# A delta-rule attention and two gated networks on one core: the inverse spread evenly, four array quadrants, spaced loads, one block

## The reference

```
attention, per batch and head:      kt = k / (|k| + 1e-6), state = 0 (48 x 48)
  for t in 0..767:                  y[t] = q[t] @ state
                                    state += beta[t] * outer(kt[t], v[t] - state.T @ kt[t])
x  = y as 3072 x 384
network 1:                          h = x @ w_in (384 x 2048)
                                    g = 0 if h <= -1, h if h >= 1, else (h + 1)^2 / 4
                                    x2 = g @ w_out (2048 x 384)
network 2:                          xn = x2 / sqrt(mean(x2^2) + 1e-6) * rms_g
                                    out = (silu(xn @ w_gate) * (xn @ w_val)) @ w_out2     (hidden width 1536)
```

## Time and profile before

| | |
|---|---|
| median of 3 runs | 1338.87 us |
| the profiled execution, its own time | 1335.86 us |
| its span, first to last instruction | 1334.1 us |
| PE busy | 1197.8 us, 90% |
| DVE busy | 608.3 us, 46% |
| ACT busy | 430.6 us, 32% |
| mean granted TensorE clock | 0.941 |
| data moved | 47.97 MB, 36 GB/s over the span |

### The profile page before, as it was taken

How to read it: one execution, slowest core, us unless ns; L and a number is a source line. 1 busy time by engine, 2 the same in 40 slices (tenths; PEclk the granted TensorE clock), 3 DMA queues, 4 the chain that set the end, 5 groups by cost and what they waited for, 6 DMA issues and landing times. The chain is left out here.

```text
span 1334.1 us, 24559 instructions
## 1 busy us (share of the span) xinstructions
PE 1197.8 (90%) x10980; PEld 959.9 (72%) x10980; DVE 608.3 (46%) x987; ACT 430.6 (32%) x709; POOL 9.6 (1%) x20
## 2 busy tenths in 40 slices
PE   2597779977998799789979999799999999999997
PEld 2376557755776577567757777688888888888886
DVE  3912860468258625942792244544233232423322
ACT  2333332223433433243234345452222323222211
POOL 1000000000000000000000000000000000000000
PEclk8878975988999899999999999899999999999999
DMA  7604000130022004100100022220101001010101
GB/s 192 142 3 97 0 1 1 27 94 1 2 50 71 2 2 73 47 2 2 49 24 2 2 93 73 75 91 0 48 0 48 0 24 24 0 24 0 24 0 24
DMA packets 18130, 47.97 MB, mean 36 GB/s; under 512 B 2224, under 2 KB 9008, under 8 KB 17456
## 3 DMA queue, kind: packets, MB, share of 16 engines
q1 hardware_dynamic: 18032, 46.51, 13.5%
HBM read 37.06 MB, written 9.44 MB: 35 GB/s over the span
## 5 line engine op out<-in xcount | busy, mean ns | idle before, releaser
L1012 DVE TENSOR_TENSOR pr<-g,vps 128x512 f32<-128x512 f32 x72 | 49.5, 688 | 252.5 <-ACT g L962 252.3
L821 PE MATMUL hps<-xh,w1h 128*128 128x512 f32 x288 | 131.7, 457 | 31.4 <-DVE g L676 31.2
L834 PE MATMUL acc<-g1h,w2h 128*128 128x512 f32 x288 | 129.3, 449 | 12.8 <-DVE g1l L683 12.8
L962 ACT ACTIVATE g<-gps 128x512 f32<-128x512 f32 x72 | 43.1, 598 | 272.3 <-PE vps L1080 272.3
L553 ACT ACTIVATE g1h<-g 128x512 fp32r<-128x512 f32 x96 | 60.6, 631 | 190.8 <-DVE g L676 168.9
L821 PE MATMUL hps<-xl,w1h 128*128 128x512 f32 x288 | 119.8, 416 | 1.6 <-issue 1.6
L821 PE MATMUL hps<-xh,w1l 128*128 128x512 f32 x288 | 119.9, 416 | 0.0
L834 PE MATMUL acc<-g1l,w2h 128*128 128x512 f32 x288 | 117.6, 408 | 0.0
L834 PE MATMUL acc<-g1h,w2l 128*128 128x512 f32 x288 | 117.1, 407 | 0.0
L683 DVE TENSOR_TENSOR g1l<-g,g1h 128x512 fp32r<-128x512 f32 x96 | 66.0, 687 | 85.0 <-ACT g1h L553 84.8
L544 ACT ACTIVATE g<-hps,half_c 128x512 f32<-128x512 f32 x96 | 65.4, 681 | 119.6 <-PE hps L821 118.6
(11 more groups left out here) (133 smaller groups left out, 2225.7 us busy)
## 6 DMA issues: line engine op xcount, KB each, us to landing
kqT<-kq SPq DMA_DIRECT2D x12, 768.0 KB, 11.2
v_in<-v SPq DMA_DIRECT2D x6, 768.0 KB, 4.3
k_in<-k SPq DMA_DIRECT2D x6, 768.0 KB, 13.1
x2d<-x2s SPq DMA_DIRECT2D x18, 256.0 KB, 2.2
x2t<-x2d SPq DMA_DIRECT2D x6, 768.0 KB, 4.3
y<-y_t SPq DMA_DIRECT2D x48, 96.0 KB, 2.2
stage<-w_in SPq DMA_DIRECT2D x4, 768.0 KB, 16.0
stage<-w_out SPq DMA_DIRECT2D x4, 768.0 KB, 4.6
```

What stands on the lines that cost most here:

```text
L821: last = pe.matmul(hps[f % 2][:, :], wt[:, kk, P * f:P * f + P], xx[:, kk, :], start=(kk == 0 and e == 0), stop=(kk == KD - 1 and e == 2))
L834: last = pe.matmul(acc[j][:, :], wt[:, f, P * j:P * j + P], gg[:, f % 2, :], start=(f == 0 and e == 0), stop=(f == NF1 - 1 and e == 2))
L962: act.activation(silu[:, f % 2, :], gps[f % 2][:, :], ACT.Silu).then_inc(e_silu, 1)
L1012: dve.tensor_tensor(pr[:, f % 2, :], silu[:, f % 2, :], vps[f % 2][:, :], ALU.mult).then_inc(e_pr, 1)
```

## The change

It changes six things. (1) The inverse: `DENSE` goes from 690 to 570, `LEAD` from 850 to 700, `GK` of the next step moves ahead of the `KS` groups, so that the inverse of the next step begins earlier in the round; the transposes `tr` and `ft` are three instead of four (one of them over all 128 partitions), and `Z` waits for the first of `ft` alone. (2) The attention's groups cover half of the instances (64 records) instead of a quarter; the small matmuls of `GK`, `GQ`, `KS`, `U`, `QS`, `PU`, `KU` go through all four 64x64 quadrants of the array in turn and write to two banks; `Y` is taken apart into `QS` and `PU`; `Z` and `X` keep their two. (3) The loads: k turned and q turned come separately, k first, and in each round v, k turned, k and q turned are issued after given blocks of network 1. (4) The first part's order: the weight pieces of network 1 are spread over the inverse one by one, and `GQ` of step 1 moves into round 1. (5) Both networks stand in one block; network 2's loops are written out; the last round also prepares network 2's first tile and 15 of its 27 weight pieces, now in single operations of 512 columns; `x2s` is copied by ACT instead of DVE. (6) The sum of squares: DVE adds the three parts (`fold`), and one fp32 matmul is left of three.

```diff
+TURNS = 3
...
 def inversion(c):
-    out = [(("tr", c, qd), 20) for qd in range(P // BLK)] + [(("nrm", c, 0), 14), (("sys", c, 0), 13)]
+    out = [(("tr", c, n), 20) for n in range(TURNS)] + [(("nrm", c, 0), 14), (("sys", c, 0), 13)]
     out += [(("inv", c, s), 4 + (BLK - 1 - s) * (s + 1) // 48) for s in range(INV)]
-    out += [(("ft", c, qd), 20) for qd in (1, 3)] + [(("xd", c, 0), 21)] + [(("ft", c, qd), 20) for qd in (0, 2)]
-    return out + [(("vn", c, 0), 17)]
+    return out + [(("ft", c, 0), 20), (("xd", c, 0), 21)] + [(("ft", c, n), 20) for n in range(1, TURNS)] + [(("vn", c, 0), 17)]
 def solve(c):
-    return [("Z", c, q) for q in range(NQ)] + [("X", c, q) for q in range(NQ)]
+    out = [(kind, c, hf) for kind in ("Z", "X") for hf in range(HALVES)]
+    if 0 < c < NSTEP - 1:
+        out += [("GK", c + 1, hf) for hf in range(HALVES)]
+    return out
 def serial(c):
-    more = c + 1 < NSTEP
-    out = []
-    for hf in range(HALVES):
-        a, b = NQH * hf, NQH * hf + 1
-        grams = [[("GK", c + 1, n)] if more else [] for n in (a, b)]
-        out += grams[0] + [("KS", c, a), ("KS", c, b)] + grams[1]
-        out += [("U", c, a), ("U", c, b), ("Y", c, a), ("KU", c, a), ("Y", c, b), ("KU", c, b)]
-    if more:
-        out += [("GQ", c + 1, n) for n in range(NQ)]
+    out = [(kind, c, hf) for hf in range(HALVES) for kind in ("KS", "U", "QS", "PU", "KU")]
+    if 0 < c < NSTEP - 1:
+        out += [("GQ", c + 1, hf) for hf in range(HALVES)]
     return out
...
-LEAD = 850
-DENSE = 690
+        if e[0] == "sys":
+            out += [("GQ", 0, hf) for hf in range(HALVES)]
+        if e[0] == "inv" and e[2] >= 2:
+            out += split(BESIDE * (e[2] - 1) // (INV - 2) - BESIDE * (e[2] - 2) // (INV - 2))
+    out += [("ft", 0, 0), ("Z", 0, 0), ("Z", 0, 1), ("xd", 0, 0)] + split(1)
+    out += [("X", 0, 0), ("X", 0, 1), ("ft", 0, 1), ("ft", 0, 2), ("vn", 0, 0), ("KS", 0, 0), ("QS", 0, 0)] + split(1)
+    out += [("mask", 0, n) for n in range(NQ)]
+    out += [("U", 0, 0), ("GK", 1, 0), ("PU", 0, 0), ("KU", 0, 0), ("GK", 1, 1)] + split(1)
+    ahead = inversion(1)
+    def some(n):
+        return [ahead.pop(0)[0] for _ in range(n)]
+    out += [("KS", 0, 1)] + split(1) + [("QS", 0, 1)] + some(1) + [("U", 0, 1)] + split(2) + some(2)
+    out += [("PU", 0, 1), ("KU", 0, 1)] + some(2) + split(1) + [("low", 0, NPIECE - 2), ("low", 0, NPIECE - 1)]
+    assert not pieces
+    return out + [("XT", 0, n) for n in range(KD)], ahead
+LEAD = 700
+DENSE = 570
 LAST = 0.90
-EDGE = 0.985
...
-        at += w / LEAD
+        at += w / (LEAD if k == 1 else DENSE)
     lead = at
+    if k == 1:
+        ev += [(0.02 + 0.04 * hf, ("GQ", 1, hf)) for hf in range(HALVES)]
     us = solve(k) + serial(k)
-    span = sum(2 if u[0] == "Y" else 1 for u in us)
-    done, begin = 0, None
-    for u in us:
-        ev.append((lead + (LAST - lead) * done / span, u))
-        done += 2 if u[0] == "Y" else 1
-        if u == ("GK", k + 1, NQ - 1):
-            begin = lead + (LAST - lead) * (done + 1) / span
+    begin = None
+    for n, u in enumerate(us):
+        ev.append((lead + (LAST - lead) * n / len(us), u))
+        if u == ("GK", k + 1, HALVES - 1):
+            begin = lead + (LAST - lead) * (n + 1) / len(us)
     rest = []
     if k + 1 < NSTEP:
         at = begin
         for e, w in inversion(k + 1):
-            if at < EDGE:
+            if at < 1:
...
+def banks():
+    out, held, at = {}, [None] * NBANK, 0
+    for u in [u for plan in PLANS for u in plan]:
+        if u in FIRST or u[0] not in WIDE + NARROW:
+            continue
+        n = 2 if u[0] in WIDE else 1
+        out[u] = [((at + j) % NBANK, held[(at + j) % NBANK]) for j in range(n)]
+        for j in range(n):
+            held[(at + j) % NBANK] = (u, j)
+        at += n
+    return out
...
+def second_network():
+    norms = {2: ["square"], 3: ["fold"], 4: ["sums", "root"], 6: ["invert"], 7: ["invert"], 8: ["scale"], 9: ["hi"], 10: ["lo"]}
+    parts = {0: (15, 17), 1: (17, 19), 2: (19, 20), 3: (20, 21), 4: (21, 22), 5: (22, 24), 6: (24, 26), 7: (26, 27)}
+    out = []
+    for n in range(NSTEP):
+        for f in range(NF2):
+            out.append(("gv", n, f))
+            if f:
+                out.append(("y", n, f - 1))
+            elif n:
+                out += [("y", n - 1, NF2 - 1), ("out", n - 1, 0)]
+            out.append(("silu", n, f))
+            if n == 0:
+                for kind in ("w2h", "w2l"):
+                    out += [(kind, n, p) for p in range(*parts.get(f, (0, 0)))]
+            if n + 1 < NSTEP:
+                out += [(kind, n + 1, int(f == 7)) for kind in norms.get(f, [])]
+    return out + [("y", NSTEP - 1, NF2 - 1), ("out", NSTEP - 1, 0)]
...
+                elif kind == "fold":
+                    dve.wait_ge(e_sq, n + 1)
+                    dve.tensor_tensor(x2sq[:, 0, :], x2sq[:, 0, :], x2sq[:, 1, :], ALU.add).then_inc(e_half, 1)
+                    dve.wait_ge(e_half, n + 1)
+                    dve.tensor_tensor(x2sq[:, 0, :], x2sq[:, 0, :], x2sq[:, 2, :], ALU.add).then_inc(e_fold, 1)
...
+                if kind == "sums":
+                    pe.wait_ge(e_fold, n + 1)
+                    if n:
+                        pe.wait_ge(e_pr, (n - 1) * NF2 + 4)
+                    pe.matmul(sums_of(n)[:, :], ones[:, :], x2sq[:, 0, :], start=True, stop=True).then_inc(e_ss, 1)
+                elif kind == "gv":
...
-                    load_kq(0)
+                    load_kq(0, (0,))
                     sp.dma_start(beta_i[:, :, :].rearrange("p c t -> p (c t)"), beta[:, :]).then_inc(s_beta, 16)
+                    sp.wait_ge(s_kq[0][0], 16 * BP)
+                    load_kq(0, (1,))
                     for n in range(NSTAGE):
                         load_w(n)
                     load_v(0)
-                    load_k(0)
                     for n in range(NSTAGE, NCHUNK):
                         load_w(n)
-                    load_kq(1)
+                    load_kq(1, (0,))
+                    load_k(0)
+                    load_kq(1, (1,))
                     sp.dma_start(gain[:, :], rms_g.rearrange("(k p) -> p k", p=P), allow_slow_non_contiguous=True).then_inc(e_gain, 16)
-                    for c in range(NSTEP):
-                        if c + 2 < NSTEP:
-                            load_kq(c + 2)
+                    def after(n, f):
+                        sp.wait_ge(s_h, NF1 * n + f + 1)
+                    for c in range(1, NSTEP):
+                        load_v(c)
+                        if c > 1:
+                            x2_store(c - 2)
                         if c + 1 < NSTEP:
-                            load_k(c + 1)
-                            load_v(c + 1)
-                        if c:
-                            x2_store(c - 1)
+                            after(c - 1, 0)
+                            load_kq(c + 1, (0,))
+                        after(c - 1, 2)
+                        load_k(c)
+                        if c + 1 < NSTEP:
+                            after(c - 1, 4)
+                            load_kq(c + 1, (1,))
+                    x2_store(NSTEP - 2)
...
-                            p0, b0 = BLK * q, BLK * (q % 2)
-                            dve.transpose(sysm[p0:p0 + BLK, :, :],
-                                          gram[p0:p0 + BLK, :, b0:b0 + BLK].rearrange("p i s -> p s i")).then_inc(s_tr, 1)
+                                if c:
+                                    dve.wait_ge(p_x, HALVES * c)
+                            else:
+                                dve.wait_ge(s_tr, TURNS * c + 1)
+                            rows = (slice(0, P), slice(BLK, C), slice(C + BLK, P))[q]
...
+                    BY_ROW_BP = ((0, 0), (1, 1), (0, 1), (1, 0))
+                    BY_ROW_M = ((0, 0), (0, 1), (1, 0), (1, 1))
+                    BY_ROW_S = ((0, 0), (0, 1), (1, 1), (1, 0))
...
                         if kind == "GK":
-                            if q == 0:
-                                pe.wait_ge(s_kq[c % 2], 16 * MEM * (c // 2 + 1))
-                            for j, i in enumerate(insts(q)):
-                                for m in range(MEM):
-                                    r = slice(C * m, C * m + D)
-                                    last = pe.matmul(ps[C * m:C * m + C, C * j:C * j + C], kqT[c % 2][r, i, 0, :],
-                                                     kqT[c % 2][r, i, 0, :], start=True, stop=True)
+                            if hf == 0:
+                                pe.wait_ge(s_kq[0][c % 2], 16 * BP * (c // 2 + 1))
+                            for h in range(H):
+                                for bp, m in BY_ROW_BP:
+                                    r, i = slice(C * bp, C * bp + D), NPAIR * hf + H * m + h
+                                    last = pe.matmul(bank_of(u, bp)[C * m:C * m + C, C * h:C * h + C], kqT[c % 2][r, 0, i, :],
```

(36 more changed lines are left out.)

766 lines of the change are left out of this document (366 added, 400 removed).

## The result

The changed kernel takes 1111.16 us (median of 4 runs, 1107.6 to 1114.05), the kernel before beside it 1340.78: ratio 0.830, 95% interval 0.8255 to 0.8345. I had predicted 1170.

The account below looks back on a forecast made before the run. PE bounds the kernel: network 2 without gaps, the rounds with waits on DVE and lost clock. First part 86, rounds 618, change of block and network 2 463.5 give 1167.5 span; forecast 1170, own range 1145 to 1195, overall 1095 to 1220.

Parts of the forecast that it names:

- Step "quadrants": Small attention matmuls: four quadrants leave a record at 29.4 ns, set by its columns of weights, so no gain.
- the other end: Same matmuls: each quadrant loads by itself, half price a record, -63 us in the rounds; first rival, 1102 us, chance 0.27.
- The rest of the rounds: Five rounds with network 1: group boundaries, GQ, sum of squares and remaining waits bring 722.4 us to 618.
- Group boundaries: Rounds: groups of 64 records instead of 32 leave out 66 boundaries of 0.33 us, -21.8 us.
- Waits left: Rounds: PE's remaining waits and lost clock, 15 us in round 1, 6 in round 2, 4 in each other, +33.
- Rival 2: Rounds: DVE works in order, so PE's waits stay, moved; 1232 us with all 95, 1200 with half; chance 0.18.
- the mark for all three: Sign in the rounds: PE's waits for g, gl and ft under 25 us together.
- The half clock of the first round: PE at half clock from about 182 to 236 us while busy; its wait for ft before Z came just before.
- The first part: Step 0's attention up to network 1's first matmul: 130.3 us falls to 86 (80 to 98).
- k alone: First part: k is loaded first, half of the bytes, so GK starts at about 7 us instead of 14.0, -7.
- `Z` and `U`: First part: Z needs only the first transpose, and U follows the inverse by 11 us instead of 21.9, -10.8.
- Change of block and network 2: After the rounds: joint falls from 13.5 to 4.2 us, sums of squares save 8.6, together 463.5.

Follow-up runs that it names:

- Experiment 2: Changed kernel with another order per kind: GK, U on one quadrant at a time, GQ, QS same-row pairs, KS, PU same-column pairs, KU diagonal pairs; 1223.87 us.
- experiment 1: Changed kernel with its small attention matmuls visiting the two quadrants of one diagonal in turn, then the other diagonal, instead of all four; 1167.24 us.
- after: The changed kernel itself, with all six changes to the kernel before; 1111.16 us.
- experiment 3: Changed kernel with the narrow-weight groups KU, Z and X on one quadrant after the other, 64-column groups still on four; 1151.38 us.
- experiment 9: Changed kernel without the fold: three matmuls of ones a tile again, no adding on DVE; 1122.8 us.
- experiment 7: Changed kernel with one tr and one ft transpose done twice and the x2s copies back on DVE; 1128.13 us.
- experiment 8: Changed kernel with Z waiting for all transposes of the inverse instead of the first; 1119.01 us.

## Why the prediction was right, and where it was wrong

**Step "quadrants": this was the error.** I took 29.4 ns a record as before, with half of it as the other end. Measured: 17.0 ns for 64 columns of weights, 13.6 for `KU`'s 48. The argument for my value was that "four add none to either side", since two already differ in rows and in columns. It took for granted that the side (rows or columns) is what a load occupies. Experiment 2 shows that it is the quadrant: pairs on the same side run like pairs on the diagonal, and a single quadrant at little over half of their rate. The trace before could not tell this, since the kernel had no group on one quadrant or on four; but my choice between the ends rested on a picture, not on a row. The price that I read, "about one cycle each" per column, was the price of two quadrants side by side, and one quadrant has it at 0.81 ns (52.0 / 64). That the columns of weights set it, not the moving columns, was right: `GK` moves 64 columns and `U` 48, and alone on a quadrant they take 3.33 and 3.29 us.

The size of the other end was off as well: -63 in the rounds, where experiment 1 against after gives -49.6. I had multiplied a full round by 5, but rounds are not alike: 58 groups of 64 columns at 1.84 - 1.09 = 0.75 are 43.5, and 10 of `KU` at 1.44 - 0.87 are 5.7, together 49.2. The 0.75 is less than half of 1.84: 3.33, 1.84 and 1.09 us fit 0.34 + 2.98 / (number of quadrants), so a group has a part of 0.34 us (2 x 1.09 - 1.84) that more quadrants do not divide. What it is, no run shows.

By the Trainium skill (TensorE: Matmul & The Clock Gate, LDWEIGHTS (loading the stationary operand)) a load takes the number of columns over 1.2, in ns: by estimate from that rule 53.3, 40 and 26.7 for 64, 48 and 32. The single quadrants of experiments 2 and 3 have 52.0, 40.5 and 31.7, so the trace agrees for 64 and 48 columns and not quite for 32. The same page (Part 3, The mechanism) says that loads overlap running matmuls only where the row group differs. The times of experiment 2 show no such difference: 1.83 us in the same rows against 1.81 in the same columns.

**The rest of the rounds: right.** With quadrants in pairs they take 601.3 where I had 618. Group boundaries were worth more than I said. 64 records in one group among network 1's matmuls take 1.84, with the boundary 1.84 + 0.33 + 0.34 - 0.47 = 2.04, two groups of 32 took 2 x 1.27: 0.50 saved at each, 33 instead of 21.8. Waits left were 33 in the sum; in experiment 1 PE is idle for 19.3 of the 601.3 us and the clock is at 0.99, another 6. So both terms erred to the dear side, 11 and 8. The 33 rested on a count of DVE's work alone.

**Rival 2, the waits that stay:** hardly any of it. Waits for `g` and `gl` are 19.5 us in after, and none is left for `ft` in the rounds; 25 had been the mark for all three.

**The half clock of the first round:** I had put the wait for `ft` just before it. The trace before has the clock at 1.00 up to 180.8 us and at 0.50 from 181.0, and the wait for `ft` from 182.7 to 186.0, behind the fall. In front of it PE was busy 1.4 of the 4 us from 176 to 180, with a wait of 2.64 us for `g`. So what stood in front of the fall are waits for `g`, not the one for `ft`.

**The first part: 86 against 89.0, and by luck.** With pairs it would be 99.6, 14 over my number. `GK` at 7.93 instead of 14.04 is the step "k alone" (-6.1 against -7). But "`Z` and `U`" failed by half: `Z` comes 2.07 us behind the inverse as said, `U` 20.0 behind it (44.80 to 64.80), where I had 11 and before had 21.9. Timeline after, PE and DVE:

```profile
44.80 1.92 DVE L924 STREAM_TRANSPOSE tt<-inv 128x1024 f32<-128x1024 f32 x1
46.87 2.21 PE L1030 MATMUL bank<-tt,gram 32*32 32x32 f32 x128 [1.11 <-DVE tt L924]
...
51.19 1.06 PE L1041 MATMUL bank<-gram,sysm 32*32 32x32 f32 x30
52.24 1.76 DVE L932 TENSOR_TENSOR v_in<-v_in,ntok 128x1536 f32<-128x1536 f32 x1
...
55.70 2.82 PE L1041 MATMUL bank<-gram,sysm 32*32 32x32 f32 x98 [3.45 <-issue]
58.45 2.17 PE L1052 MATMUL bank<-state,kqT 48*64 48x48 f32 x63
60.44 2.00 PE L1076 MATMUL hps<-state,kqT 48*64 48x48 f32 x61
60.77 1.02 DVE L952 TENSOR_TENSOR v_in<-v_in,bank 128x384 f32<-128x384 f32 x2 [6.77 <-PE bank L1052]
```

I counted DVE's operations, but DVE is done with `vn` at 54.0 and then waits 6.77 us for PE. The chain is PE's: `X` stands behind a weight piece (49.02 to 51.19, while ACT is done with the copies of `Z` at 50.51), pauses 3.45 us in the midst of a group, and `X`, `KS` and `QS` run at half clock, with a second weight piece (62.37 to 64.80) in front of `U`. A step that counts one engine's work on a path has to look for the others that stand in it. `U` to the first `hps` matmul was 24.2 where I had 27.

**Change of block and network 2: right.** 465.1 against 463.5; `gps` follows at once, each tile has one sum (experiment 9: 11.6 us for six tiles against 10.2).

**Spread.** The prediction had no term of its own for it. It is worth 19.4 us in the new kernel and nothing that can be measured in the old one. Waits and clock of before, 118 us in the rounds, are some 25 in after (20 of idle time, 5 of clock). Of these 93 us the spread has some 20, DVE's lighter load 13 to 20 (experiment 7) and the early `Z` 3 to 5 (experiment 8), if the three add. The remainder is about half. The new order of the groups and the halves are what is left to bring it, but I did not separate them: its cause is open.

## What to carry to other kernels

Small float32 matmuls on one engine are paid by their columns of weights and nearly divided by the number of quadrants that are visited in turn (3.33, 1.84 and 1.09 us), so here the order of visits alone was worth 41% of each group. Where a price is open between "shared" and "separate", and no row has a lone user of the resource, neither end has a row for it: give them like chances, or look for a row with one user. Here an evener schedule brought 19 us in one kernel and nothing measurable in the other, where the clock was lower, so count the granted clock with the waits; an operation that may wait for a load belongs behind the others in its engine's queue.

## What the hardware showed that I had not expected

64 float32 records with their weight loads (32 matmuls of the program, two records each), in us from the first to the next matmul behind them, at the full clock:

| columns of weights | one quadrant | two | four |
|---|---|---|---|
| 64 | 3.33 | 1.84 (rows 1.83, columns 1.81) | 1.09 |
| 48 | 2.59 | 1.44 | 0.87 |
| 32 | 2.03 | 1.13 | not run |

Each row with three values fits a fixed part and a part that is divided by the number of quadrants: 0.34 + 2.98 / n for 64 columns, 0.30 + 2.30 / n for 48.

Four quadrants bring a record to 17.0 and 13.6 ns. The Trainium skill (TensorE: Matmul & The Clock Gate, Back-to-back issue gap) has some 25 ns as the least distance from one matmul to the next; counted by records the groups on four quadrants are under it, counted by matmuls of the program (34 and 27 ns) they are not.

In the first part the clock fell to its lower level (1.2 GHz) and stayed there while PE was busy:

```profile
44.80:52.24 7.44, 6.33 (x164) 3.88 (x163) 7.37 (x5) 2.95 (x5) 0.00 (x0) 0.80 1.04 224
52.24:55.70 3.46, 0.01 (x1) 0.00 (x0) 1.76 (x1) 0.00 (x0) 0.95 (x1) 0.50 0.95 147
55.70:64.80 9.10, 9.10 (x230) 7.31 (x229) 3.43 (x6) 4.43 (x6) 0.00 (x0) 0.50 0.06 6
```

Cut finer, it was 1.00 up to 49.3 us and 0.50 from 49.4. In front of the fall PE had waited 1.11 us and then run `Z` (46.87 to 49.02); in experiment 8, where PE had no work from 45.8 to 52.18, it fell between 49.5 and 49.8. So the pause in `X` (52.24 to 55.70) came behind the fall and is not its cause. Behind the pause PE was busy without a gap, and the clock rose at 66.4, in the midst of `U`. `KS` and `QS` took some 2.0 us each at the lower level, four quadrants notwithstanding, against 1.08 at the full clock: what the quadrants gain, the lower level takes away again. The pause itself ("issue") remains open. It lies at a time when the DMA engines are 0.95 busy, and it is not there in experiment 8, in which `X` starts at 58.16; no kernel here took the loads away from it.
